# Attention scores of two heads: one zero-padded matmul, or two 64-row matmuls

## The chip, the cores and the metric

The program runs on one core of a Trainium2 chip. The metric is the device time of one execution in microseconds (us), less is better. TensorE (PE) multiplies, VectorE (DVE), ScalarE (ACT) and GpSimd (POOL) work elementwise, and SyncE (SP) issues the DMAs. TensorE writes into PSUM, which has eight banks of 512 fp32 columns.

## What is computed

Windowed attention with a distance bias, then a dense block with a squared ReLU, then a mixture of eight experts whose gate goes through eight rounds of normalisation. The part that the change touches is the first product of the attention; cut down:

```
q, k, v: (4, 8, 576, 64)                      # batch, heads, sequence, head size
scores = q @ k.T / 8                          # 64 values are summed for each score
mask: 0 <= query - key < 128
scores = where(mask, scores - slope[head] * distance, -1e9)
attn = exp(scores - max); attn /= sum + 1e-9
x = attn @ v                                  # to (2304, 512)
x = relu(x @ w_in) ** 2 @ w_out               # 512 -> 2048 -> 512
P = balanced(exp(x @ w_gate))                 # (2304, 8)
out = sum over e of P[:, e] * (relu(x @ w1[e]) @ w2[e])
```

## The kernel before

The engines run programs of their own and wait for each other through semaphores; no scheduler orders the work. The order is a list of events that every engine's program walks through (`alone_events`, L287, and `window_events`, L300). The program has four stages.

- **Ahead of the loop** the attention of batch 0 runs alone. Here all tiles that two steps share are doubled (n = 2), and q and k stay in fp32 (`plain`).
- **The loop** has three passes. Pass w computes the dense block of batch w and, between its matmuls, the attention of batch w + 1. The dense block is cut into 64 groups: eight rounds of four groups of layer 1 (L636, mostly 12 matmuls each) and four of layer 2 (L643; the first has 21 matmuls, the second 3, the others 12). Here q and k are split into a high and a low fp32r part, and a score is the sum of three products (n = 1).
- Then the dense block of batch 3 without attention, and then the experts (L704 and L760).

A batch's attention takes the heads in four pairs (c = 0 to 3). Of a pair, 576 positions make four tiles of 128 and a tail of 64, so that a batch has 4 x 5 = 20 steps. One **slot** holds step j's scores (`scores`, L601), the transposes of step j - 2's probabilities (`transpose_p`, L612) and the product of step j - 3 with the values (`attend`, L627). A query tile needs its own key tile and the one before it; only the first of a pair (t = 0) has one key tile. In the loop slot j stands behind group 2 * (4 + j + j // 5) + 1.

Before a pair's scores, its k and q have to lie with the head's 64 values on the partitions. That is done in three **rounds** (`transpose_round`, L563): round 0 transposes four tiles of k (L572), round 1 four tiles of q, round 2 both tails (L576). All write bank 3 (t_ps). ACT copies the bank out (`round_hi`, L824; in the loop this is the high part), then DVE (`round_lo`, L1003; in the loop the low part), which adds to the semaphore t_lo, for which the next round waits. The two heads of a pair fill partitions 0 to 63 and 64 to 127. The keys (kzh, kzl, and kz0 ahead of the loop) are kept twice as wide, one half for each head, with zeros on the other head's partitions. So one matmul with all 128 rows and 2 x 256 columns gives both heads' scores, in one bank (s_ps: bank 0, and 4 where n = 2). DVE reads them from there (`biased`, L1028), adds the bias, and notes the negative maximum; that raises neg_done, after which the bank is free. ACT takes the exponentials (L854), DVE divides by the sums (L1065), and only then can slot j + 2 transpose them.

In the loop the rounds of pair 0 stand behind groups 3, 5 and 8, those of the next pairs behind the group n of slot 4, 9 or 14 (behind that slot), n + 2 and n + 5. SP loads a pair's k and q when the transposes of the pair before are done.

## Time and profile before

| | |
|---|---|
| median of 3 runs | 2166.37 us (2164.35 to 2172.43) |
| the profiled execution | 2173.03 us |
| its span, first to last instruction | 2171.2 us |
| TensorE busy with matmuls | 2113.9 us (97% of the span) |
| VectorE, ScalarE, GpSimd busy | 1362.2, 588.7, 976.9 us |
| ahead of the loop | 0 to 70.5 us |
| the three passes | 70.5 to 219.9, to 367.7, to 512.4 us |
| dense block of batch 3 | to 634.4 us |
| experts | to the end |

A row of the profile names the line, the engine and the instruction, then what it writes and what it reads, with the shape as rows * columns of the array, then partitions x elements. The ends of matmuls are modelled: of a single matmul the duration includes its way through the array, so two that follow each other overlap in the rows. What a matmul costs is read from the distance between two starts. Where a row stands for several instructions (x4), its duration runs from the first start to the last end. "idle before <- who" is the time in which the engine stood still and what released it.

### The profile page before, as it was taken

To read this page: it belongs to the slowest core of one execution; us is meant where nothing else is said; L and a number is where in the kernel's file an instruction comes from. 1 tells how busy PE (TensorE), PEld (TensorE's weight loads), DVE (VectorE), ACT (ScalarE), POOL (GpSimd) and SP (SyncE) were. 2 spreads that over 40 slices of the span, in tenths; PEclk is the share of its full clock that TensorE was granted. 3 is DMA by queue.
4 is the path that set the end of the run, shared out by engine and by line. 5 is a ranking of instruction groups with operands and counts; after the bars stand their busy time and mean duration, and the time that the engine had idled before them with its cause. 6 is when DMAs were issued, how large, how long until landed. Compare 5 with 4: busy or idle time off the path is not lost.

```text
span 2171.2 us, 39510 instructions
## 1 busy us (share of the span) xinstructions
PE 2113.9 (97%) x13270; PEld 1909.8 (88%) x13270; DVE 1362.2 (63%) x3012; ACT 588.7 (27%) x1609; POOL 976.9 (45%) x680
## 2 busy tenths in 40 slices
PE   7899999999899899999999999999999999999999
PEld 4799898889888799899899899889989989989988
DVE  7566675675556766666666666666666666666665
ACT  5565564564421121111111111211111111111111
POOL 3122222224444354554554554665455455455451
PEclk9999999999999999999999999999999999999999
DMA  5232333322210111111111111112111111111111
GB/s 124 63 82 65 93 87 82 87 71 74 69 49 30 39 40 49 40 49 48 39 48 43 43 48 39 48 41 91 50 39 48 48 39 48 43 44 48 39 48 53
DMA packets 165123, 121.05 MB, mean 56 GB/s; under 512 B 64400, under 2 KB 129936, under 8 KB 165008
## 3 DMA queue, kind: packets, MB, share of 16 engines
q1 hardware_dynamic: 165008, 119.59, 19.4%
q8 instruction: 63, 1.03, 0.2%
q14 instruction: 52, 0.43, 0.1%
HBM read 114.84 MB, written 4.72 MB: 55 GB/s over the span
## 4 chain that ended last, share of the span: by engine, by line
PE 91%; DVE 6%; ACT 2%; issue 2%; DMA 0%; SPq 0%; DVEq 0%; ACTq 0%
PE bank L760 35%; PE bank L704 33%; PE bank L643 9%; PE bank L636 8%; PE bank L601 2%; PE bank L627 1%; PE bank L612 1%; DVE g1l L1077 1%; DVE relu L1108 1%; DVE xl L1091 1%; DVE row L1142 1%; ACT prob L854 1%; PE bank L572 0%; DVE acc L1219 0%; DVE prob L1065 0%
## 5 line engine op out<-in xcount | busy, mean ns | idle before, releaser
L1226 DVE SCALAR_TENSOR_TENSOR acc<-bank,gate,acc 128x512 f32<-128x512 f32 x531 | 398.5, 751 | 285.5 <-PE bank L760 283.6
L704 PE MATMUL bank<-xh,eh 128*128 128x288 f32 x1792 | 532.2, 297 | 0.5 <-DVE u L1192 0.5
L704 PE MATMUL bank<-xl,eh 128*128 128x288 f32 x1792 | 530.7, 296 | 0.0
L704 PE MATMUL bank<-xh,el 128*128 128x288 f32 x1792 | 528.6, 295 | 0.0
L760 PE MATMUL bank<-fh,gh 128*128 128x512 f32 x1152 | 450.9, 391 | 0.7 <-DVE acc L1219 0.4
L760 PE MATMUL bank<-fh,gl 128*128 128x512 f32 x1152 | 450.7, 391 | 0.0
L760 PE MATMUL bank<-fl,gh 128*128 128x512 f32 x1152 | 450.6, 391 | 0.0
L704 PEld LDWEIGHTS bank<-xh,eh 128*128 128x128 f32 x1792 | 338.0, 189 | 3.3 <-DVE u L1192 0.7
L704 PEld LDWEIGHTS bank<-xl,eh 128*128 128x128 f32 x1792 | 338.2, 189 | 2.6
L704 PEld LDWEIGHTS bank<-xh,el 128*128 128x128 f32 x1792 | 339.1, 189 | 0.0
L483 POOL TENSOR_TENSOR wl<-stage,wh 128x512 fp32r<-128x512 f32 x120 | 159.1, 1326 | 380.1 <-ACT wh L822 380.1
L529 POOL TENSOR_TENSOR ew<-a,ew 128x256 f32<-128x256 f32 x64 | 47.3, 740 | 507.6 <-DMA ew<-in_moe_w_dram 489.5
L1184 DVE SCALAR_TENSOR_TENSOR gl<-bank,gh 128x288 fp32r<-128x288 f32 x512 | 220.8, 452 | 76.4 <-ACT gh L941 61.0
L822 ACT ACTIVATE p<-bank 128x288 f32<-128x288 f32 x128 | 52.3, 409 | 784.5 <-PE bank L704 784.5
L538 POOL TENSOR_TENSOR el<-ew,eh 128x1792 fp32r<-128x1792 f32 x64 | 259.6, 4056 | 11.5 <-POOL eh L536 11.5
L760 PEld LDWEIGHTS bank<-fh,gl 128*128 128x128 f32 x1152 | 216.9, 188 | 45.8
L760 PEld LDWEIGHTS bank<-fh,gh 128*128 128x128 f32 x1152 | 216.8, 188 | 45.4 <-DVE acc L1226 0.9
L760 PEld LDWEIGHTS bank<-fl,gh 128*128 128x128 f32 x1152 | 216.9, 188 | 43.5
L636 PE MATMUL bank<-xr,wh 128*128 (+1 forms) x1024 | 213.2, 302 | 4.7 <-issue 3.7
L636 PEld LDWEIGHTS bank<-xr,wh 128*128 128x128 f32 x1024 | 166.3, 191 | 9.1 <-issue 8.3
L643 PE MATMUL bank<-g1h,wh 128*128 128x288 f32 x512 | 160.1, 313 | 14.6 <-DVE g1l L1077 14.5
L542 POOL TENSOR_TENSOR fl<-fw,fh 128x1024 fp32r<-128x1024 f32 x64 | 154.9, 2420 | 11.5 <-POOL fh L540 11.5
(128 smaller groups left out, 2987.9 us busy)
## 6 DMA issues: line engine op xcount, KB each, us to landing
fw<-in_moe_w_dram SPq DMA_DIRECT2D x64, 512.0 KB, 3.6
stage<-in_moe_w_in_dram SPq DMA_DIRECT2D x64, 256.0 KB, 3.0
stage<-in_moe_w_out_dram SPq DMA_DIRECT2D x64, 256.0 KB, 2.7
ew<-in_moe_w_dram SPq DMA_DIRECT2D x64, 256.0 KB, 2.8
a<-in_moe_w_dram SPq DMA_DIRECT2D x64, 128.0 KB, 2.6
ew<-in_moe_w_dram SPq DMA_DIRECT2D x64, 128.0 KB, 2.8
k_raw<-in_k_dram SPq DMA_DIRECT2D x32, 128.0 KB, 2.6
q_raw<-in_q_dram SPq DMA_DIRECT2D x32, 128.0 KB, 2.5
```

The source lines that it names most:

```text
L483: pool.tensor_tensor(wl[s][:, i, :], stage[:, i % 2, :], f(wh[s][:, i, :]), ALU.subtract).then_inc(w_split, 1)
L529: pool.tensor_tensor(raw[:, S1, :, :], a21[r][:, :, :], raw[:, A22, :, :], ALU.add).then_inc(e_chain, 1)
L538: pool.tensor_tensor(el[r][:, :, :, :], raw[:, :, :, :], low, ALU.subtract).then_inc(e_split, 1)
L542: pool.tensor_tensor(fl[r][:, :, :], fw[r][:, :, :], f(fh[r][:, :, :]), ALU.subtract).then_inc(f_split, 1)
L601: last = pe.matmul(o, x[:, t * P:(t + 1) * P], y[:, :, n0:(t + 1) * P], start=(i == 0), stop=(i == len(products) - 1))
L636: last = pe.matmul(ps[:, 0:nt], w[s][:, kc, c * P:(c + 1) * P], xx[:, kc, at], start=(kc == 0 and w is wh and xx is hi), stop=(kc == KC - ...
L643: last = pe.matmul(ys[m % len(ys)][:, 0:BH], w[s][:, KC + c, m * P:(m + 1) * P], x[:, c, :], start=(c == 0 and w is wh and x is g1h), stop ...
L704: done = pe.matmul(ps[:, 0:BH], w[r][:, a, kc, :], x[:, j, b, kc, :], start=(first and kc == 0 and w is eh and x is xh), stop=(kc == 1 and ...
L760: done = pe.matmul(z_ps[t % 3][:, :], x[:, c, at], w[r][:, c, :], start=(c == 0 and x is ghf and w is fh), stop=(c == 1 and x is glf))
L822: return act.activation(o, i, ACT.Copy, scale=scale)
L1184: return dve.scalar_tensor_tensor(out=gl[:, f2, j, n2, :], in0=ps, scalar=0.0, in1=f(gh[:, f2, j, n2, :]), op0=ALU.max, op1=ALU.subtract)
L1226: dve.scalar_tensor_tensor(out=z, in0=ps, scalar=weight, in1=z, op0=ALU.mult, op1=ALU.add).then_inc(z_free, 1)
```

## The change

The keys are kept once (kTh, kTl, kT0), each head on its own 64 partitions and without zeros. A score product becomes two matmuls that read 64 partitions each, one a head, with half as many columns. They write two banks: ahead of the loop banks 0 and 4 for head 0 and banks 6 and 7 for head 1, in the loop bank 0 and bank 3. Bank 3 is also the one that the rounds write, so in the loop a round has to wait until DVE has read the scores of head 1 (neg_done), and the rounds stand in other places: behind groups 3, 5 and 7 for pair 0, and behind n + 1, n + 2 and n + 5 for the others. The scores of slot 0 wait for three rounds, those of a later pair's first tile for two and of its second tile (before: its fifth) for all three. Copies of k go over 128 partitions in one instruction. Ahead of the loop ACT alone copies k out, DVE only steps the semaphore; the clearing of the padded keys goes.

```diff
-        kz0 = sb("kz0", [P, 2, 2, QT * P], fp32, placed["qT0"])
+        kT0 = sb("kT0", [P, 2, QT * P], fp32, placed["qT0"])
...
-        kzh = sb("kzh", [P, 2, QT * P], fp32r, placed["qTl"])
-        kzl = sb("kzl", [P, 2, QT * P], fp32r, placed["kzh"])
-        v_sb = sb("v_sb", [P, 2, QT, 2 * D], fp32, placed["kzl"])
+        kTh = sb("kTh", [P, QT * P], fp32r, placed["qTl"])
+        kTl = sb("kTl", [P, QT * P], fp32r, placed["kTh"])
+        v_sb = sb("v_sb", [P, 2, QT, 2 * D], fp32, placed["kTl"])
...
-        s_ps, pT_ps = [bank[0], bank[4]], [bank[1], bank[5]]
+        pT_ps = [bank[1], bank[5]]
         o_ps, t_ps = bank[2], bank[3]
...
+        def s_ps(j, n, h):
+            if h == 0:
+                return bank[4 * (j % n)][:, 0:2 * P]
+            return bank[3 if n == 1 else 6 + j % 2][:, 0:2 * P]
...
             after = {n: [] for n in range(len(groups))}
-            apart = (0, 2, 5)
+            apart = (1, 2, 5)
             if with_attention:
                 for r in range(ROUNDS):
-                    after[3 + apart[r]].append(("round", 0, r))
+                    after[3 + 2 * r].append(("round", 0, r))
                 after[0] += [("v", 0), ("v", 1)]
...
             pool.memset(ones[:, :], 1.0).then_inc(ones_ready, 1)
-            for z in (kzh[:], kzl[:], qTh[:, FULL * P:], qTl[:, FULL * P:]):
+            for z in (kTh[:, FULL * P:], kTl[:, FULL * P:], qTh[:, FULL * P:], qTl[:, FULL * P:]):
                 pool.memset(f(z), 0.0).then_inc(zeros_later, 1)
...
             pe.wait_ge(ident_ready, 1)
-            pe.wait_ge(zeros_ready, 3)
-            def transpose_round(b, c, r):
+            pe.wait_ge(zeros_ready, 2)
+            def transpose_round(b, c, r, before=0):
                 if r < 2:
...
                     wait_alone(pe, t_lo, b * (ROUNDS * KC) + (ROUNDS * c + r))
+                    if plain(b):
+                        pe.wait_ge(t_hi, ROUNDS * c + r)
+                if before:
+                    wait_alone(pe, neg_done, b * STEPS + before)
                 if r < 2:
...
                 if t == 0:
-                    pe.wait_ge(t_lo, b * (ROUNDS * KC) + ROUNDS * c + 2)
-                if t == FULL:
+                    pe.wait_ge(t_lo, b * (ROUNDS * KC) + ROUNDS * c + (2 if n > 1 or c else 3))
+                if t == (FULL if n > 1 else 1):
                     pe.wait_ge(t_lo, b * (ROUNDS * KC) + ROUNDS * (c + 1))
+                if plain(b) and t in (0, FULL):
+                    pe.wait_ge(t_hi, ROUNDS * c + (2 if t == 0 else 3))
                 bank_wait(neg_done, b, j, n)
-                o = s_ps[j % n][:, :].rearrange("p (h k) -> p h k", h=2)[:, :, k0:]
                 n0 = (t - 1) * P + k0
                 if plain(b):
-                    products = ((qT0[:, s, :], kz0[:, s, :, :]),)
+                    products = ((qT0[:, s, :], kT0[:, s, :]),)
                 else:
-                    products = ((qTh, kzh), (qTh, kzl), (qTl, kzh))
+                    products = ((qTh, kTh), (qTh, kTl), (qTl, kTh))
                 for i, (x, y) in enumerate(products):
-                    last = pe.matmul(o, x[:, t * P:(t + 1) * P], y[:, :, n0:(t + 1) * P],
-                                     start=(i == 0), stop=(i == len(products) - 1))
+                    for h in range(2):
+                        d = slice(h * D, (h + 1) * D)
+                        last = pe.matmul(s_ps(j, n, h)[:, k0:], x[d, t * P:(t + 1) * P], y[d, n0:(t + 1) * P],
+                                         start=(i == 0), stop=(i == len(products) - 1))
                 last.then_inc(s_done, 1)
...
                     if what == "round":
-                        transpose_round(b, *a)
+                        transpose_round(b, *a, 0 if n > 1 or a[0] == 0 else a[0] * QT + (a[1] == 2))
                     if what == "slot":
...
                 s = c % n
+                act.wait_ge(t_done, b * (ROUNDS * KC) + (ROUNDS * c + r + 1))
                 if plain(b):
-                    act.wait_ge(t_done, b * (ROUNDS * KC) + (ROUNDS * c + r + 1))
                     if r == 1:
                         act.sem_inc(t_hi, 1)
-                        return
-                    o, i = (slice(0, FULL * P), slice(0, FULL * P)) if r == 0 else (slice(FULL * P, S), slice(TAIL, 2 * TAIL))
-                    for h in range(2 if r else 1):
-                        d = slice(h * D, (h + 1) * D)
-                        last = copy(kz0[d, s, h, o], t_ps[d, i])
-                    last.then_inc(t_hi, 1)
+                    elif r == 0:
+                        copy(kT0[:, s, 0:FULL * P], t_ps[:, :]).then_inc(t_hi, 1)
+                    else:
+                        copy(kT0[:, s, FULL * P:S], t_ps[:, TAIL:2 * TAIL]).then_inc(t_hi, 1)
                     return
-                act.wait_ge(t_done, b * (ROUNDS * KC) + (ROUNDS * c + r + 1))
-                if r == 1:
+                if r == 0:
+                    last = copy(kTh[:, 0:FULL * P], t_ps[:, :])
+                elif r == 1:
                     last = copy(qTh[:, 0:FULL * P], t_ps[:, :], SCALE)
-                if r == 2:
+                else:
                     copy(qTh[:, FULL * P:S], t_ps[:, 0:TAIL], SCALE)
-                if r != 1:
-                    o, i = (slice(0, FULL * P), slice(0, FULL * P)) if r == 0 else (slice(FULL * P, S), slice(TAIL, 2 * TAIL))
-                    for h in range(2):
-                        last = copy(kzh[h * D:(h + 1) * D, h, o], t_ps[h * D:(h + 1) * D, i])
+                    last = copy(kTh[:, FULL * P:S], t_ps[:, TAIL:2 * TAIL])
                 last.then_inc(t_hi, 1)
...
             dve.memset(qT0[:, :, FULL * P:], 0.0).then_inc(zeros_ready, 1)
-            for r in range(2):
-                dve.memset(kz0[:, r, :, :], 0.0).then_inc(zeros_ready, 1)
+            dve.memset(kT0[:, :, FULL * P:], 0.0).then_inc(zeros_ready, 1)
             dve.wait_ge(dist_ready, 1)
...
-                    dve.wait_ge(t_done if r == 1 else t_hi, b * (ROUNDS * KC) + (ROUNDS * c + r + 1))
                     if r == 0:
-                        last = dve.tensor_copy(kz0[D:2 * D, s, 1, 0:FULL * P], t_ps[D:2 * D, :])
-                    else:
-                        at = slice(0, FULL * P) if r == 1 else slice(FULL * P, S)
-                        last = dve.tensor_scalar(qT0[:, s, at], t_ps[:, 0:FULL * P if r == 1 else TAIL],
-                                                 SCALE, None, ALU.mult)
-                    last.then_inc(t_lo, 1)
+                        dve.sem_inc(t_lo, 1)
+                        return
+                    dve.wait_ge(t_done if r == 1 else t_hi, ROUNDS * c + r + 1)
+                    at = slice(0, FULL * P) if r == 1 else slice(FULL * P, S)
+                    dve.tensor_scalar(qT0[:, s, at], t_ps[:, 0:FULL * P if r == 1 else TAIL],
+                                      SCALE, None, ALU.mult).then_inc(t_lo, 1)
                     return
                 dve.wait_ge(t_hi, b * (ROUNDS * KC) + (ROUNDS * c + r + 1))
-                if r == 1:
+                if r == 0:
+                    last = lo(kTl[:, 0:FULL * P], t_ps[:, :], kTh[:, 0:FULL * P])
+                elif r == 1:
                     last = lo(qTl[:, 0:FULL * P], t_ps[:, :], qTh[:, 0:FULL * P], SCALE)
-                if r == 2:
+                else:
                     lo(qTl[:, FULL * P:S], t_ps[:, 0:TAIL], qTh[:, FULL * P:S], SCALE)
-                if r != 1:
-                    o, i = (slice(0, FULL * P), slice(0, FULL * P)) if r == 0 else (slice(FULL * P, S), slice(TAIL, 2 * TAIL))
-                    for h in range(2):
-                        d = slice(h * D, (h + 1) * D)
-                        last = lo(kzl[d, h, o], t_ps[d, i], kzh[d, h, o])
+                    last = lo(kTl[:, FULL * P:S], t_ps[:, TAIL:2 * TAIL], kTh[:, FULL * P:S])
                 last.then_inc(t_lo, 1)
...
                 last = dve.tensor_tensor_reduce(
-                    out=prob[0:nq, j % 2, h, k0:], in0=s_ps[j % n][0:nq, h * 2 * P + k0:(h + 1) * 2 * P],
+                    out=prob[0:nq, j % 2, h, k0:], in0=s_ps(j, n, h)[0:nq, k0:],
                     in1=bias[0:nq, 2 * (j // QT) + h, k0:], scale=-1.0, scalar=3.0e38,
...
```

The instruction streams, at three places. TensorE in the loop, slot 1, the scores and the transposes behind them. Before:

```order
L601 MATMUL bank<-kzh,qTh 128x512 [waits neg_done]
L601 MATMUL bank<-kzl,qTh 128x512
L601 MATMUL bank<-kzh,qTl 128x512
L612 MATMUL bank<-ident,prob 128x128 [waits pT_out,norm_done]
L612 MATMUL bank<-ident,prob 128x128 x3
```

Of the change:

```order
L615 MATMUL bank<-kTh,qTh 128x256 [waits neg_done]
L615 MATMUL bank<-kTh,qTh 128x256
L615 MATMUL bank<-kTl,qTh 128x256 x2
L615 MATMUL bank<-kTh,qTl 128x256 x2
L626 MATMUL bank<-ident,prob 128x128 [waits pT_out,norm_done]
L626 MATMUL bank<-ident,prob 128x128 x3
```

Three matmuls of 512 columns have become six of 256, the two heads in turn.

TensorE in the loop, around the first round of pair 1 (k_raw; q_raw is the second round's). Before:

```order
L627 MATMUL bank<-pT,v_sb 64x128 [waits x_lo,pT_out]
L627 MATMUL bank<-pT,v_sb 64x128 x3
L565 REGISTER_ALU
L572 MATMUL bank<-ident,k_raw 128x128 [waits k_in,t_lo]
L572 MATMUL bank<-ident,k_raw 128x128 x3
L666 REGISTER_ALU
L636 MATMUL bank<-xr,wh_51 128x288 [waits relu_done]
```

Of the change:

```order
L650 MATMUL bank<-xr,wl_53 128x288
L572 REGISTER_ALU
L268 REGISTER_ALU [waits k_in,t_lo]
L583 MATMUL bank<-ident,k_raw 128x128 [waits neg_done]
L583 MATMUL bank<-ident,k_raw 128x128 x3
L680 REGISTER_ALU
L650 MATMUL bank<-xr,wh_51 128x288 [waits relu_done]
```

The transposes of k have moved from behind slot 4's product with the values to behind the layer-1 group that follows; the transposes of q stay where they were, one group on.

DVE at the start of the program. Before:

```order
L989 MEMSET qT_55 128x2x128
L991 MEMSET kz_56 128x1280 x2
L994 TENSOR_SCALAR bias<-prob 128x256 [waits dist_ready]
L994 TENSOR_SCALAR bias<-prob 128x256 x7
L1009 COPY kz_56<-bank 64x512 [waits bias_ready,t_hi]
L1012 TENSOR_SCALAR qT_55<-bank 128x512 [waits t_done]
```

Of the change:

```order
L999 MEMSET qT_55 128x2x128
L1000 MEMSET kT_56 128x2x128
L1003 TENSOR_SCALAR bias<-prob 128x256 [waits dist_ready]
L1003 TENSOR_SCALAR bias<-prob 128x256 x7
L1021 TENSOR_SCALAR qT_55<-bank 128x512 [waits bias_ready,t_done]
```

Two clearings of 1280 columns have become one of 256, and the copy of k is no longer DVE's.

## Rows read from the trace of the kernel before

**Rows 1.** The page's chain of work that ended last, shares by engine.
```profile
PE 91%; DVE 6%; ACT 2%; issue 2%; DMA 0%; SPq 0%; DVEq 0%; ACTq 0%
```

**Rows 2.** Stretches: window, length, busy us (instructions) of each engine, clock, DMA.
```profile
0.00:70.50 70.50, 50.20 (x296) 28.00 (x296) 49.80 (x203) 39.93 (x133) 19.96 (x32) 0.97 0.41 97
...
219.90:367.70 147.80, 144.28 (x1084) 132.26 (x1084) 95.06 (x300) 82.40 (x240) 42.18 (x32) 0.99 0.32 82
```

**Rows 3.** Timeline (start, duration, engine, line, instruction) of TensorE, a wide slot in the loop.
```profile
252.63 0.40 PE L601 MATMUL bank<-kzl,qTh 128*128 128x512 f32 x1
252.86 0.39 PE L601 MATMUL bank<-kzh,qTl 128*128 128x512 f32 x1
...
253.99 0.53 PE L636 MATMUL bank<-xr,wh 128*128 x2
254.36 0.29 PE L636 MATMUL bank<-xr,wl 128*128 x1
254.49 0.43 PE L636 MATMUL bank<-xr,wh 128*128 x2
```

**Rows 4.** Timeline of TensorE, a slot whose transposes have 64 rows.
```profile
301.46 0.39 PE L601 MATMUL bank<-kzh,qTl 128*128 128x512 f32 x1
301.78 0.46 PE L612 MATMUL bank<-ident,prob 64*128 64x64 f32 x4
```

**Rows 5.** Timeline of TensorE, a narrow slot (one key tile).
```profile
266.83 0.28 PE L601 MATMUL bank<-kzh,qTh 128*128 128x256 f32 x1
266.95 0.28 PE L601 MATMUL bank<-kzl,qTh 128*128 128x256 f32 x1
```

**Rows 6.** Timeline of TensorE, the gate's matmuls on four column tiles.
```profile
645.52 4.09 PE L777 MATMUL bank<-acc,wgz 128*32 128x288 f32 x64
```

**Rows 7.** Timeline of all engines, rounds 0 and 1 of a pass's first pair.
```profile
229.85 1.18 ACT L822 ACTIVATE kzh<-bank 64x512 fp32r<-64x512 f32 x2
...
231.06 1.39 DVE L1001 SCALAR_TENSOR_TENSOR kzl<-bank,kzh 64x512 fp32r<-64x512 f32 x2 [0.63 <-ACT kzh L822]
...
231.44 0.29 PE L643 MATMUL bank<-g1h,wl 128*128 128x288 f32 x1
...
232.60 0.63 PE L572 MATMUL bank<-ident,q_raw 128*128 128x128 f32 x4 [0.86 <-DVE kzl L1001]
```

**Rows 8.** Timeline of all engines, rounds 0 and 1 of the second pair (pair 1).
```profile
259.06 0.66 PE L572 MATMUL bank<-ident,k_raw 128*128 128x128 f32 x4
...
261.33 0.41 ACT L917 ACTIVATE relu<-bank 128x288 f32<-128x288 f32 x1 [0.38 <-PE bank L636]
...
261.97 0.62 ACT L822 ACTIVATE wh<-stage 128x512 fp32r<-128x512 f32 x1
...
262.71 0.60 PE L572 MATMUL bank<-ident,q_raw 128*128 128x128 f32 x4
...
265.13 0.40 PE L643 MATMUL bank<-g1h,wh 128*128 128x288 f32 x1 [0.23 <-DVE g1l L1077]
```

**Rows 9.** Timeline of DVE, round 2 of the third pair (pair 2).
```profile
301.02 0.45 DVE L1001 SCALAR_TENSOR_TENSOR kzl<-bank,kzh 64x64 fp32r<-64x64 f32 x2
```

**Rows 10.** Line L994 (ns min/median/max), and the timeline of all engines, near the start.
```profile
L994 DVE TENSOR_SCALAR bias<-prob x8: 273/279/2023, 3.7 to 7.1; 128x256 f32<-128x256 f32 x8
...
8.29 1.09 PE L572 MATMUL bank<-ident,q_raw 128*128 128x128 f32 x4 [2.40 <-DVE kz L1009]
...
8.94 0.60 SPq L360 DMA_DIRECT2D v_sb<-in_v_dram  x1
```

**Rows 11.** Chain of waits ahead of the loop: start, length, what.
```profile
10.81 0.37 SPq L358
...
15.37 1.71 PE bank L601 x2
...
26.09 1.05 PE bank L601 x2
...
49.19 2.00 PE bank L601 x2
```

## The prediction

> **What bounds the kernel now.** I read the chain of waits first: 91% of it is TensorE [rows 1]. Then the stretches: in one pass of the loop that holds the attention (three passes) TensorE is busy for 144.28 of 147.80 us, in the stage ahead of the loop for 50.20 of 70.50 [rows 2]. So in the loop each TensorE start that moves later costs its own length. Ahead of it, DVE, ACT and TensorE take turns, and only what is on their chain counts. The change touches nothing after the third pass: at most some 512 of 2171 us are in play.
>
> **Score matmuls in the loop.** A slot has three matmuls of 512 columns, 0.23 apart (252.63 to 252.86), 0.70 in all [rows 3]; where a query tile has one key tile they have 256 columns and are 0.12 apart, 0.36 in all [rows 5]. Afterwards there are six of 64 rows and half as many columns, for two heads in turn. The trace of before has no such pair. The nearest rows are matmuls on different column tiles: 64 of 288 columns take 4.09, 0.06 each [rows 6], against 0.13 for one 288-column matmul on the whole array (254.36 to 254.49 [rows 3]), so several run at once. I take it that row tiles overlap in the same way: a pair of 256 columns then takes 0.12, as one such matmul does now.
>
> Against that stand two changes of tiling in each slot. (a) The change itself: from the third 128-row score matmul to the first 64-row transpose 0.32 pass, not 0.23 [rows 4]: 0.09. (b) The first weight load behind a change isn't hidden: behind the column-tiled matmuls of attend the first two 128-row matmuls take 0.37 (253.99 to 254.36), two later ones would take 2 x 0.13: 0.11 [rows 3]. Into transposes it is less: four take 0.66 behind attend and 0.60 behind a layer-1 matmul [rows 8]: 0.06. By these:
> - a wide slot followed by 128-row transposes (12 in a pass): 0.09 + 0.11 + 3 x 0.12 + 0.09 + 0.06 = 0.71 for 0.70, so +0.01 each;
> - the three wide slots whose transposes have 64 rows themselves: no way out is paid, and the way in that the old code paid (0.09 and about 0.05) goes: 0.56 for 0.84, -0.28 each;
> - the narrow slots: 128 columns stream in about 0.06, less than the load (0.11), which sets the pace: 0.09 + 0.11 + 2 x 0.11 + 0.06 + 0.15 = 0.63 for 0.36, +0.27, three times, and +0.34 for slot 0, which is followed by a layer matmul; slot 1 for the same reason +0.06.
> Sum of a pass: 0.12 - 0.84 + 0.81 + 0.34 + 0.06 = +0.5; three passes **+1.5 us**. Halving the streamed columns is paid back by drains and loads.
>
> The Trainium skill (TensorE: Matmul & The Clock Gate, Part 3, table of measured speed-ups) gives 3.07 for four row tiles, less than four. As an estimate from that page, a pair would keep 77% of the overlap, which adds some 5 us to the sum; no run here shows it.
>
> **Copies of the keys, and the rounds, in the loop.** A round's key copy falls from two 64-partition instructions each on ACT (1.18) and DVE (1.39) to one each, half of that [rows 7].
> - First pair of a pass: ACT starts at 229.85, would be done at 230.45, and DVE, free by then, at 231.2 (half of 1.18 and of 1.39). TensorE's matmul of 231.44 is followed 0.13 later by the transposes of q, at 231.57, and not at 232.60, where they wait for that copy [rows 7]: -1.03, three times, **-3.1**.
> - Pairs 1 and 3: the transposes of k now come one layer-1 group later (bank 3 holds head 1's scores until DVE has read them) and those of q stay, so one group of some 1.6 us lies between them, not two. Queued ahead on ACT are that group's relu and the copy of a square (0.64 from 261.33 to 261.97) and a weight copy (0.62) [rows 8]. From 259.06 the group's 12 matmuls take 0.24 + 10 x 0.13, and k's last transpose starts at about 261.1. Then: relu at 260.95, the weight copy done at 262.2, key copy to 262.7, DVE's part to 263.45, transposes of q at 263.6 where TensorE could have started them at 262.8. That is a new stall of 0.8. TensorE's wait ahead of 265.13, 0.23 idle for a square that DVE delivers late [rows 8], then goes, because the stall comes before it. Net 0.8 - 0.23, so about +0.5, six times: **+3.0**. Bounds: 0 (ACT serves the copy at once) and +0.8 each.
> - Pair 2: groups of layer 2 give ACT less to do; +0.1. The third round has to be copied one slot sooner (the wait moved from tile 4 to tile 1). In pair 2 DVE's part ends at 301.47 now [rows 9], 0.25 sooner with one copy fewer on ACT and DVE, while the scores started at 300.99, two starts of 0.23 before the row of 301.46 [rows 4]: +0.2 to +0.3. In pairs 1 and 3 ACT has no relu there and I count nothing. Leaving the transposes of k between two layer groups and not behind attend costs 0.05 a round (one more unhidden load of 0.11, one of 0.06 saved). Together +0.45 a pass, **+1.3**.
> - The new waits for head 1's scores (round 0 and round 2) find them read: DVE reads within a microsecond, the group between takes 1.6. Nothing; if not, up to 0.5 each, 18 times, which is a rival below.
> Loop: +1.5 - 3.1 + 3.0 + 1.3 = **+2.7**.
>
> **Ahead of the loop.** DVE no longer clears 2 x 1280 columns and POOL clears two times 1280 fewer, which it now does while DVE's first bias instruction takes 2.02, where the median is 0.28 [rows 10]. DVE's copy of k (some 0.7, as half of the 1.39 [rows 7]) is gone too. Both stand ahead of q's transposes at 8.29 [rows 10]: by 1.7 + 0.7 they could start some 2 us sooner, once q has landed. But the next loads of k are issued by SP behind those of v, whose last issue starts at 8.94 and takes 0.60 [rows 10]; the k load is issued at 10.81 now [rows 11] and can go to 9.54, so it moves by 1.27 at most. I take -1.25. The second matmul pair behind it is on the chain with 1.71 [rows 11]: half of the columns and the two changes of tiling, -0.3. Another stands there with 2.00, about twice the 1.05 of the one at 26.09 [rows 11], so at the lower of the two levels: -0.5. In three places scores are on the chain with that 1.05, and DVE's normalised tile is next to be late: 0 to -0.3 each, I take -0.15. ACT's tail copy is one instruction and not two: -0.2. Sum -1.25 - 0.3 - 0.5 - 0.45 - 0.2 = **-2.7**; bounds -1 and -5. Elsewhere the chain there runs over DVE, ACT and the transposes, and faster scores only wait longer.
>
> **Sum.** +2.7 - 2.7 = 0.0. The profiled run took 2173.03 (span 2171.2), the median is 2166.37; the terms are differences and carry over: **2166 us**. About 0.5% (11 us) is what a measurement of this kernel can tell from no change.
>
> **Rivals.**
> 1. *Row tiles do not overlap.* Six matmuls of 0.12 then take 0.72 in a wide slot, +0.36, in 48 slots +17; narrow slots have six loads of 0.11, +0.33, 12 times +4; ahead of the loop +2. 2166 + 23 = **2189**, slower. It decides at 0.17 for a pair instead of 0.12. Against it: column tiles overlap fully [rows 6]. For it: no row shows two row tiles at once.
> 2. *Loads inside the row-tiled stretch are not hidden.* Each later pair costs 0.11 more: 2 x 0.11 x 48 = +10, **2176**. The Trainium skill (TensorE: Matmul & The Clock Gate, Part 3, what overlaps and what doesn't) says a load overlaps running matmuls only where its row group differs. Against it speaks the row of four 64-row transposes, all on one row group, in 0.46 [rows 4], where loads in the open would add to each.
> 3. *The copies get in the way*: the new waits for scores in bank 3 and for the third round bind (0.5 in 18 rounds), the stall of pairs 1 and 3 is 1.3 and not 0.8: +9 + 3, **2178**. For it: DVE is busy for 95.06 of 147.80 [rows 2] and serves in order. Against it: the layer groups give it 1.6 us.
> 4. *Entering and leaving cost nothing here*, because the two row tiles drain one behind the other's back: -0.35 in 57 slots, -20, with -4 ahead of the loop for the clock kept up: **2144**, faster. Against it: [rows 4] is a change into 64 rows and has the 0.09.
> 5. *The change does not do what it says* (the 64-row form is executed as full 128 rows, each matmul alone): the same as rival 1.
>
> **Chances.** Forecast 0.66 (2158 to 2173: the stalls at their bounds, the start between -1 and -5, and a stretch of lower clock more or less at a loop boundary). Rival 1 and 5 together 0.13, rival 2 0.06, rival 3 0.06, rival 4, whole or in part, 0.09. The range 2157 to 2180 leaves out rival 1 and most of rival 4. Faster by over 0.5% (under 2155.5) 0.10, slower (over 2177.2) 0.16, within 0.74.
>
> **What would show it.** Score matmuls in pairs that start within 0.01 of each other, pairs 0.12 apart, and some 0.09 more before the first and behind the last; if all six are 0.12 apart, rival 1 holds. No wait in front of the transposes of q in a pass's first pair; one of about 0.8 in pairs 1 and 3. Transposes of q before 7.1 at the start, the loop from about 67.8 instead of 70.5, passes about 1 us longer than now. I am wrong if pairs lie much closer than 0.12, if the 0.11 for the load is missing, or if the rounds wait for neg_done.

## The result, and the profile after

The changed kernel takes **2171.8 us** (median of 20 executions, 2168.5 to 2175.6) where the kernel before takes 2166.7 (2163.0 to 2172.4): ratio 1.0022, 95% interval 1.0013 to 1.0030, so 4.9 us more (2.8 to 6.5). The forecast was 2166.0, no difference. The time lies within the range, but the difference is real, and it is a loss. (A ratio, here and below, compares with executions of the kernel before that were taken beside it. It isn't the quotient of the two medians: in run 6 it is 1.0033 where the medians give 1.0016.) The profiled execution took 2173.73 us with a span of 2171.7, nearly the 2171.2 of before; one profile of each, laid side by side, doesn't show where the time is.

Most of what the forecast said of the rows came true. The chain of waits is still TensorE's:

```profile
PE 92%; DVE 5%; ACT 1%; issue 1%; SPq 0%; DMA 0%; DVEq 0%; ACTq 0%
```

A wide slot in the loop (timeline of TensorE; a row of x2 is one pair, head 0 and head 1), beside [rows 3]:

```profile
251.10 0.29 PE L657 MATMUL bank<-g1h,wl 128*128 128x288 f32 x1
251.33 0.38 PE L615 MATMUL bank<-kTh,qTh 64*128 64x256 f32 x2
251.55 0.28 PE L615 MATMUL bank<-kTl,qTh 64*128 64x256 f32 x2
251.67 0.28 PE L615 MATMUL bank<-kTh,qTl 64*128 64x256 f32 x2
251.88 0.66 PE L626 MATMUL bank<-ident,prob 128*128 128x128 f32 x4
```

Two row tiles run at once: in a row of x2 they start some 0.005 apart, and the third pair follows the second after 0.12, as one 256-column matmul did. Ahead of the first pair stand 0.23 instead of 0.13 (the change of tiling), behind it 0.22 (the load in the open), behind the last 0.21. Slots with 64-row transposes and narrow slots, beside [rows 4, 5]:

```profile
301.13 0.39 PE L615 MATMUL bank<-kTh,qTh 64*128 64x256 f32 x2
301.32 0.32 PE L615 MATMUL bank<-kTl,qTh 64*128 64x256 f32 x2
301.44 0.31 PE L615 MATMUL bank<-kTh,qTl 64*128 64x256 f32 x2
301.56 0.40 PE L626 MATMUL bank<-ident,prob 64*128 64x64 f32 x4
...
266.31 0.33 PE L615 MATMUL bank<-kTh,qTh 64*128 64x128 f32 x2
266.48 0.27 PE L615 MATMUL bank<-kTl,qTh 64*128 64x128 f32 x2
266.59 0.28 PE L615 MATMUL bank<-kTh,qTl 64*128 64x128 f32 x2
266.79 0.66 PE L626 MATMUL bank<-ident,prob 128*128 128x128 f32 x4
```

From a 64-row pair into 64-row transposes only 0.12 pass: no way out is paid. The rounds, beside [rows 7, 8]. In pair 0 (the first five rows) the transposes of q follow without a wait. In pair 1 ACT has a relu, a square and a weight copy ahead of the key copy; DVE is done at 262.28, and TensorE waits 0.80 for it:

```profile
229.38 0.58 ACT L836 ACTIVATE kTh<-bank 128x512 fp32r<-128x512 f32 x1
229.99 0.69 DVE L1010 SCALAR_TENSOR_TENSOR kTl<-bank,kTh 128x512 fp32r<-128x512 f32 x1
...
231.12 0.60 PE L583 MATMUL bank<-ident,q_raw 128*128 128x128 f32 x4
...
259.61 0.60 PE L583 MATMUL bank<-ident,k_raw 128*128 128x128 f32 x4
...
260.44 0.62 ACT L836 ACTIVATE wh<-stage 128x512 fp32r<-128x512 f32 x1
...
260.96 0.59 ACT L836 ACTIVATE kTh<-bank 128x512 fp32r<-128x512 f32 x1
...
261.59 0.69 DVE L1010 SCALAR_TENSOR_TENSOR kTl<-bank,kTh 128x512 fp32r<-128x512 f32 x1 [0.51 <-ACT kTh L836]
...
262.57 0.63 PE L583 MATMUL bank<-ident,q_raw 128*128 128x128 f32 x4 [0.80 <-DVE kTl L1010]
```

The start (timeline of all engines), beside [rows 10, 11]. DVE's first bias instruction no longer stretches to 2.02 (line L1003 has a maximum of 0.841), so q's transposes start at 6.40 and not at 8.29. But k of the next pair is issued only at 9.67 to 10.77, behind v, and its transposes wait 3.30 for it; in before they start at 14.29. Of 1.9 us won, 0.8 are left:

```profile
6.40 1.09 PE L583 MATMUL bank<-ident,q_raw 128*128 128x128 f32 x4 [0.88 <-DMA q_raw<-in_q_dram]
...
8.94 0.60 SPq L366 DMA_DIRECT2D v_sb<-in_v_dram  x1
...
9.67 1.06 SPq L364 DMA_DIRECT2D k_raw<-in_k_dram  x2
...
10.77 0.60 SPq L366 DMA_DIRECT2D k_raw<-in_k_dram  x1
...
13.50 1.09 PE L583 MATMUL bank<-ident,k_raw 128*128 128x128 f32 x4 [3.30 <-DMA k_raw<-in_k_dram]
```

The stretches, beside [rows 2]. The granted clock is the third figure from the end, here 0.90, 0.80 and 1.00; 1.00 is the upper level (2.4 GHz), half of it the lower one:

```profile
0.00:70.80 70.80, 49.56 (x336) 31.47 (x336) 42.72 (x198) 39.23 (x129) 18.04 (x32) 0.90 0.41 97
27.00:78.00 51.00, 39.96 (x291) 28.11 (x288) 30.36 (x143) 29.99 (x101) 10.67 (x11) 0.80 0.28 71
220.90:368.10 147.20, 143.11 (x1144) 129.50 (x1144) 90.05 (x292) 78.98 (x232) 41.62 (x32) 1.00 0.32 83
```

The loop starts at 70.83, not at 67.8; ahead of it the clock is 0.90, where before has 0.97.

Both figures are too high. The trace of before has its first record of the clock at 18.4, that of the change at 25.8, and the view counts 1.00 until then, though the matmuls run at the lower level. Four transposes of probabilities, in the chain of waits of before, then of the change:

```profile
20.16 0.65 PE bank L612 x4
```
```profile
25.00 1.02 PE bank L626 x4
```

So of the time ahead of the loop the change spends 40 us at the lower level (25.8, and 14.3 of the later stretches) and before 23 (18.4 and 4.3).

### The profile page after: what moved, and what is told of

Same layout as the page of the kernel before. It is cut to its first block, busy times and chain, and to the rows that moved or that the text cites. A ratio compares the mean times of both kernels' runs of the same rounds, so it can differ in the third digit from the quotient of the medians.

```text
span 2171.7 us, 39932 instructions
## 1 busy us (share of the span) xinstructions
PE 2114.6 (97%) x13490; PEld 1909.6 (88%) x13490; DVE 1342.1 (62%) x2983; ACT 577.7 (27%) x1581; POOL 973.4 (45%) x680
## 4 chain that ended last, share of the span: by engine, by line
PE 92%; DVE 5%; ACT 1%; issue 1%; SPq 0%; DMA 0%; DVEq 0%; ACTq 0%
PE bank L774 35%; PE bank L718 33%; PE bank L657 9%; PE bank L650 9%; PE bank L641 2%; PE bank L626 2%; PE bank L615 2%; DVE xl L1097 1%; DVE row L1148 1%; PE bank L583 1%; DVE relu L1114 1%; DVE g1l L1083 0%; DVE prob L1041 0%; ACT prob L864 0%; DVE acc L1225 0%
```

## Experiments

**Theory A.** The new loop costs what the forecast says. Ahead of it the 64-row scores leave TensorE idle for longer, the granted clock falls more often, and that takes back the earlier start. **Rivals:** all of the loss is in the loop (B); the earlier start lowers the clock (C).

Loop starts and pass lengths below are read from the first layer-1 matmul of each pass. A mean clock is the mean over all executions of a kernel of the granted clock of each; a clock of a stretch, and the microseconds at the lower level, are those of the one profiled execution.

**1. Ahead of the loop alone** (`ahead_only`): as after, but in the loop

```diff
-                    products = ((qTh, kTh), (qTh, kTl), (qTl, kTh))
+                    products = ((qTh, kzh), (qTh, kzl), (qTl, kzh))
...
-            apart = (1, 2, 5)
+            apart = (0, 2, 5)
```

with the copies, waits, bank and clearing of before. Expected:

> Only the stage ahead of the loop is changed (64-row score matmuls, keys unpadded, ACT alone copies k); the loop keeps the padded keys, the 128-row matmuls and the old places of the rounds. Theory A (the shorter score matmuls leave TensorE idle for more of this stage, so it is granted the lower clock for longer, and that takes back what the earlier start gave): in the trace of the changed kernel 40 of the first 71 us are at the lower level, in that of before 23, and the loop starts at 70.8 as against 70.5; so 0 to +3 us against the kernel before, and a loop start at 70 to 73. Rival B (the forecast's sum for this stage was right, and all of the loss is in the loop): -2.7 us, loop start at about 68.

Measured: 2166.03, ratio 0.9996 (0.9987 to 1.0005), so -0.9 us (-2.8 to +1.1). That is below A's 0 to +3, and the interval excludes neither A nor B's -2.7. The loop start, 72.07, is as A says. It is the profile with the lowest clock ahead of the loop, 0.76 from 27 to 78 us:

```profile
27.00:78.00 51.00, 41.77 (x292) 28.57 (x291) 31.93 (x141) 30.06 (x102) 10.63 (x11) 0.76 0.27 67
```

Since the sum with the next run didn't come to 4.9, it was run again:

> The change ahead of the loop alone, once more and on another chip. Its first result does not add up with the others: the new loop costs 0.75 a pass (2.3) in every profile, the whole change 4.9, so the part ahead of the loop should cost some 2.6, but it measured 2166.03 against 2167.49. Theory A (its low clock is a matter of chance from execution to execution, more often than with the old scores): this time clock 0.989 to 0.990 and 2168 to 2170, and in the profile again 13 us or more at the lower level before 78 us. Rival (with the old loop behind it the stage is better off, and the clock of the whole change has a second cause in the loop): 0.991 and 2165.5 to 2166.5 again.

Measured: 2168.16, ratio 1.0000 (0.9991 to 1.0009), loop start 69.19, 0.87 from 27 to 78. The mean clock of its executions is 0.9907 (first run 0.9908), between the 0.9926 of before and the 0.9893 of the change. A's time (2168 to 2170) and its 13 us at the lower level (13.7) were met, its clock (0.989 to 0.990) was not; of the rival, the clock was met and the time was not. So the stage alone brings nothing that can be measured (-0.9 and 0.0 us; -2.7 is outside the second interval), and with the new loop behind it the clock is a little lower still.

**2. The loop alone** (`loop_only`): as after, but ahead of the loop the padded `kz0`, its clearing and copies, and

```diff
-                    products = ((qT0[:, s, :], kT0[:, s, :]),)
+                    pe.matmul(o, qT0[:, s, t * P:(t + 1) * P], kz0[:, s, :, n0:(t + 1) * P],
+                              start=True, stop=True).then_inc(s_done, 1)
```

> Only the loop is changed; the stage ahead of it keeps padded keys, their clearing, and one 128-row score matmul a step. Theory A: the loop costs what the forecast's sum for it says, +2.7 us, since passes 2 and 3 in the trace of the changed kernel are 1.1 (with the one stretch of lower clock of before at 219.8 taken out) and 0.7 us longer than before, and the stage ahead +2. Rival B: the loop costs the whole +4.9, above all through its new wait for the transposes of q in pairs 1 and 3 (0.93 instead of 0.8, six times) and something that the two traces do not show; then +4.5 to +5.

Measured: 2169.03, ratio 1.0006 (0.9997 to 1.0015), mean clock 0.9924 as before. A's +2.7 lies within the interval (-0.6 to +3.3); B's +4.5 is out. The passes settle it. These are the ones that run wholly at the upper level, without those of `apart135` (other places of the rounds) and of `after_fill` (run 3); one of the five at 145.25 is `apart025`:

| | old loop | new loop |
|---|---|---|
| pass 1 | 146.56 | 147.29, 147.33 |
| pass 2 | 146.39, 146.42, 146.48, 146.53, 146.65 | 146.99, 147.25, 147.46, 147.47 |
| pass 3 | 144.49 to 144.53 (6 profiles) | 145.25 to 145.26 (5 profiles) |

So some 0.75 a pass, 2.3 us in three.

**3. More work for TensorE, as added instructions** (`after_fill`):

```diff
+                if plain(b):
+                    for i in range(4):
+                        pe.transpose(pT_ps[j % n][:, i % 4 * P:(i % 4 + 1) * P], ident[:, :], ident[:, :])
                 wait_alone(pe, norm_done, b * STEPS + (j + 1))
```

> The changed kernel, and ahead of the loop four more 128x128 transposes of the identity in each step, into the bank that the step's own transposes overwrite, just before TensorE waits for the normalised probabilities: work without use where it stands idle for 1.0 to 1.7 us in each step. Theory A (idle time ahead of the loop costs clock): the stage ends earlier, loop start at 67 to 69 instead of 70.8, 2 to 4 us less than the changed kernel, about 2168 where the kernel before takes 2166.7. Rival B (the clock there plays no part): the extra work is hidden at best, 2172, and later where it sticks out, up to 0.2 in each of 20 steps, 2176.

Measured: 2175.95, ratio 1.0043 (1.0029 to 1.0056), the time of B. Clock and loop start do what A says (1.00 from 27 to 78, mean clock 0.9920, loop start 68.59), but this kernel doesn't test A's price: passes 2 and 3 last 151.99 and 149.48, 4.7 and 4.2 more than in after, though nothing in the loop was changed (at these two boundaries it is also at the lower level for 6.8 and 3.4 us). At both boundaries a second wait (2.23 and 2.42) stands behind the first, without a releaser in the profile; the boundary at 216:

```profile
216.17 0.40 PE L653 MATMUL bank<-xr,wh 128*128 x1 [2.11 <-issue]
218.80 0.61 PE L653 MATMUL bank<-xr,wh 128*128 x1 [2.23 <-issue]
```

160 more TensorE instructions (80 transposes and their loads) moved the loop's code; that this is the cause is my guess and wasn't tried. The next experiment keeps the number of instructions.

**4. The same work, no instruction more** (`after_wide`):

```diff
+                        if plain(b):
+                            full = bank[4 * (j % n) if h == 0 else 6 + j % 2]
+                            last = pe.matmul(full[:, :].rearrange("p (r k) -> p r k", r=2)[:, :, k0:],
+                                             x[d, t * P:(t + 1) * P],
+                                             y[d, n0:(t + 1) * P].unsqueeze(1).to_broadcast([D, 2, (t + 1) * P - n0]),
+                                             start=True, stop=True)
+                            continue
```

(`plain` holds ahead of the loop only; each trace has 336 matmuls ahead of the loop.) 

> The changed kernel, but ahead of the loop each 64-row score matmul streams its keys twice (512 columns into the whole bank, the second 256 never read), so TensorE is as long at the scores as with padded keys, with not one instruction more or less. Theory A (what the change loses is TensorE's clock ahead of the loop, because TensorE has less to do there): mean granted clock back from 0.989 to 0.992 or more, at most 10 us at the lower level before 77 us instead of 20 to 31, loop start at 66 to 69, and 2167 to 2169 instead of 2171.8, although each step has 0.25 more work. Rival B (the clock is lower for another reason, such as the earlier start or the phase of the loads): clock 0.989 as before, and the extra columns cost 0.3 to 1 us: 2172 to 2173.

Measured: 2168.84, ratio 1.0012 (1.0003 to 1.0021); mean clock 0.9922, loop start 68.22. A holds in every number, B in none. **TensorE streams twice the columns at these scores, and the kernel takes 1.5 and 2.9 us less than the two medians of the change.** The intervals of the ratios overlap, but the means of the executions (2168.8 against 2171.5 and 2171.8) differ by 2.7 with a standard error of 0.6 from the first, and the clock goes with them. The clock from 27 to 78, this kernel, then before (its second profile, below):

```profile
27.00:78.00 51.00, 41.49 (x305) 26.78 (x301) 32.33 (x142) 31.13 (x102) 11.39 (x12) 0.93 0.31 79
```
```profile
27.00:78.00 51.00, 42.29 (x285) 27.58 (x285) 32.94 (x147) 32.07 (x107) 11.49 (x12) 0.93 0.33 81
```

**5. The same with the old loop** (`ahead_wide_oldloop`, the edits of 1 and 4):

> The same twice-streamed scores ahead of the loop, with the old loop (padded keys, 128-row matmuls, old places of the rounds). Theory A with the loop's cost of 0.75 a pass (pass 3 at full clock: 144.50 and 144.53 with the old loop, 145.25 and 145.26 with the new): 2.3 us less than the run above, and 2 us less than the change ahead of the loop alone (2166.0), so 2163 to 2165, below both kernels. Rival B: 2166.5, clock 0.991.

Measured: 2165.18, ratio 0.9999 (0.9989 to 1.0008), mean clock 0.9927, loop start 68.38. The median is 0.2 above A's band and 3.7 below run 4, but against before it shows no gain; the clock is A's, not B's 0.991.

**6. The change once more, and before once more** (`after_again`, `before_again`; no edit):

> The changed kernel once more, on the chip of the runs beside it. Theory A: median 2171 to 2173, mean granted clock 0.989 to 0.990 over its executions where the kernel before shows 0.992 to 0.993, its span at an equal granted clock within 1 us of that of before, and in this second profile again 15 us or more at the lower level before 77 us. Rival B (the loss is time at full clock, and the low clock of the first profile was chance): the same clock as the kernel before and still 4 to 5 us more.

> The kernel before, for a second profile. Theory A: less than 15 us at the lower level before 77 us (10.2 in the first one, 20 to 31 in three profiles with short scores ahead of the loop); pass 3 at full clock 144.5. Rival (the stretches are chance and not the kernel's): 20 us or more.

Measured: after 2170.38, ratio 1.0033 (1.0019 to 1.0046), mean clock 0.9894 beside 0.9929 of before on that chip. The median is 0.6 below A's band; clock and lower level (17 us between 33.7 and 50.7) are A's. The loop starts at 69.92. Before: 0.93 from 27 to 78 (6.8 us at the lower level), **loop start 68.33, not 70.54**, pass 3 144.50; both are A's. The profile that the forecast was made from was itself a late one.

**7. The rounds' places.** `apart025` puts k's transposes back behind the slot; `apart135` puts q's one group later, with (1, 3, 5) in this line:

```diff
-            apart = (1, 2, 5)
+            apart = (0, 2, 5)
```

> The changed kernel, but the transposes of k of pairs 1 to 3 back in their old place directly behind the slot (one layer-1 group earlier), now behind a wait for head 1's scores in bank 3. If the new stall of 0.93 in front of the transposes of q (six times) is what the loop's loss is made of: it goes, -0.8 x 6, less a wait for DVE behind attend that I put at 0 to 0.4 nine times (the slot's transposes and attend take 1.2 us, about what DVE needs for both heads' scores), so 2167 to 2170 and the loop's loss of some 2.5 us is gone. Rival: DVE is later than that (it has the group's squares queued ahead), and the wait behind the slot costs as much as the stall: 2171 to 2173.

> The changed kernel, but the transposes of q of pairs 1 to 3 one layer group later (n + 3), so that two groups lie between them and those of k, as before. Theory A (one group of 1.6 us is too short for ACT's and DVE's copy): the wait of 0.93 in front of them goes, but the pair's first scores now follow one group behind q's transposes and wait for q's copy instead, 0.4 to 0.9; pass 3 between 144.7 and 145.3, total 2169.5 to 2172. Rival: the copies of q fit into that group, the wait is gone altogether, pass 3 at 143.7 to 144.2 and the total at 2167 to 2168.5: then the change's loss in the loop is the placement alone, and the 64-row matmuls gain there.

Measured: `apart025` 2171.64, ratio 1.0018 (1.0009 to 1.0028), pass 3 145.25, the same as in after to 0.01; I expected 2167 to 2170. The wait only moved, to k's transposes behind attend, three times a pass:

```profile
406.42 0.63 PE L583 MATMUL bank<-ident,k_raw 128*128 128x128 f32 x4 [0.64 <-DVE negmax L1041]
```

My 0 to 0.4 for it was low; the rival held. `apart135`: 2175.47, ratio 1.0049 (1.0035 to 1.0063), slower than both and outside both expectations. The pair's first scores now wait for q's copy, 1.1 in pairs 1 and 3, where my 0.4 to 0.9 was low, and 0.3 in pair 2:

```profile
414.32 0.33 PE L615 MATMUL bank<-kTh,qTh 64*128 64x128 f32 x2 [1.11 <-DVE qTl L1010]
...
443.70 0.33 PE L615 MATMUL bank<-kTh,qTh 64*128 64x128 f32 x2 [0.30 <-DVE qTl L1010]
```

So the places of the change are the best of these three; with bank 3 shared, one of the two waits has to be paid.

**8. The earlier start** (`after_slowclear`):

```diff
-            for z in (kTh[:, FULL * P:], kTl[:, FULL * P:], qTh[:, FULL * P:], qTl[:, FULL * P:]):
+            for z in (kTh[:], kTl[:], qTh[:], qTl[:]):
```

> The changed kernel, but POOL clears all 640 columns of kTh, kTl, qTh and qTl (2560 in all, about what the kernel before clears) and not 128 of each. It delays DVE's biases and with them q's first transposes, which start at 6.40 in the changed kernel and at 7.60 where the loop (and so the clearing) is the old one. It asks why the granted clock of the changed kernel (0.989) is lower than with the change ahead of the loop alone (0.991). Theory C (the earlier first transposes leave TensorE idle longer until the next k lands at 13.5, and that starts the stage on the lower level): q's transposes at 7.6, those of pair 1's k still at 13.5, mean clock back to 0.991, median 2169 to 2170. Rival (the start plays no part; only the shorter scores do): the same 0.989, 2170 to 2172, and the earlier start was worth nothing either way.

Measured: 2172.69, ratio 1.0026 (1.0016 to 1.0036), mean clock 0.9888: the clock of the rival, the time 0.7 above it. q's transposes start at 7.52, those of k at 13.56 (after: 13.50). C falls: the start plays no part in the clock, and the first 1.1 us of the earlier start were worth 0.06.

**9. A try at a faster kernel** (`wide_tail_oldloop`: run 5, and in the last three steps ahead of the loop)

```diff
+                if plain(b) and j >= STEPS - 3:
+                    pe.matmul(pT_ps[j % n][:, :].rearrange("p (r k) -> p r k", r=4), ident[:, :],
+                              ident[:, :].unsqueeze(1).to_broadcast([P, 4, P]), start=True, stop=True)
```

> The 64-row scores ahead of the loop streaming their keys twice, the old loop, and in the last three steps ahead of the loop one more 512-column matmul of the identity before TensorE waits for the normalised probabilities. In both kernels with twice-streamed scores TensorE falls to the lower level at 67, as the attention of batch 0 runs out, and 5.2 to 5.5 us of that lie in the first pass. Theory A: with the idle time of 62 to 67 filled, this stretch goes or is halved: first pass 146.4 to 147.7 instead of 148.96, clock 0.993 to 0.994, total 2163 to 2165 where the kernel before takes 2166.9. Rival: waits of 1.2 and 1.4 between the last products with the values remain and decide it: no change, 2165 to 2166.

Measured: 2166.21, ratio 0.9994 (0.9985 to 1.0002). In the profile the lower level from 67 on is gone, as A said, and pass 1 takes 146.56:

```profile
27.00:78.00 51.00, 44.84 (x333) 28.10 (x332) 33.49 (x146) 33.28 (x106) 11.97 (x12) 1.00 0.34 86
```

The mean clock is 0.9936, the highest of all, but the median missed A's 2163 to 2165 by 1.2; a gain over before isn't shown.

**All profiles together.** Scores "short" are single 64-row pairs ahead of the loop, "long" those of before or streamed twice:

| profile | scores | clock 27 to 78 | loop start |
|---|---|---|---|
| after, after_again | short | 0.80, 0.83 | 70.83, 69.92 |
| ahead_only, again | short | 0.76, 0.87 | 72.07, 69.19 |
| apart025, apart135, after_slowclear | short | 0.83, 0.87, 0.87 | 70.66, 68.42, 68.97 |
| before, before_again | long | 0.90, 0.93 | 70.54, 68.33 |
| loop_only, after_wide | long | 1.00, 0.93 | 67.13, 68.22 |
| ahead_wide_oldloop, wide_tail_oldloop | long | 0.93, 1.00 | 68.38, 67.93 |

Every short clock is below every long one; the loop starts overlap. The means are 0.83 and 0.95 (17 and 5 us at the lower level), the mean loop starts 70.0 and 68.4. `after_fill`, short scores with the added work of run 3, has 1.00 and 68.59. The first rise to the upper level comes between 16.6 and 26.5 with short scores and between 17.4 and 19.1 with long ones; no granted clock given here counts what is lost before it.

**All executions together.** Over 216 executions of all these kernels a straight line with one slope and a level for each kernel gives 1.34 us for each 0.001 of mean clock (standard error 0.07). At an equal clock the change, both runs together, then lies 0.1 above before (standard error 0.4), which is A's expectation in run 6; `ahead_only`, both runs, 2.3 below (0.35), `loop_only` 1.3 above (0.4), `after_wide` 1.1 above (0.4). This is read from scatter and not from an edit, and a microsecond at the lower level need not cost the same in each stage (with the slope of `ahead_only` itself, 0.9, its 2.3 are some 1.5).

## Why the prediction was wrong

**Right: the loop, in most of its terms to a few hundredths.** Set against `ahead_only` in pass 3, where both run at the upper level, each slot and round measures (forecast in brackets): wide slot followed by 128-row transposes 0.00 (+0.01), narrow slot +0.27 (+0.27), slot 0 +0.32 (+0.34), slot 1 +0.06 (+0.06), slot with 64-row transposes -0.24 to -0.30 (-0.28), pair 0 -1.00 (-1.03), a moved k round +0.05 (+0.05), pair 2's wait +0.24 (+0.1). The sum was 0.9 a pass and is 0.75: 2.3 us against 2.7.

In pairs 1 and 3 the net is the forecast's +0.5 by luck. The new stall measures +0.97 from start to start (0.8), and the wait for a late square that goes in exchange is worth 0.45 (0.23). Both forecasts took the idle time of a row, and the starts move by more than that. The wait that goes, as it stands in `ahead_only` (starts 0.52 and 0.24 apart, where 0.13 is the rule):

```profile
409.66 0.29 PE L665 MATMUL bank<-g1h,wl 128*128 128x288 f32 x1
410.18 0.40 PE L665 MATMUL bank<-g1h,wh 128*128 128x288 f32 x1 [0.23 <-DVE g1l L1094]
410.42 0.30 PE L665 MATMUL bank<-g1l,wh 128*128 128x288 f32 x1
```

(The prediction also rounds 0.8 - 0.23 down to 0.5, and its sum for rival 4 comes to 2142, not 2144; neither changes the verdict.) Of the +0.2 to +0.3 for the third round of pair 2 some 0.05 is there: the slot that would wait for it gives -0.24, the two like it -0.29 and -0.30.

**Rivals 1, 2, 4 and 5** are out by the rows of the wide slot: pairs overlap whole, their loads are hidden after the first (0.12 between the second and the third pair), and entering and leaving cost 0.1 each. The estimate from the Trainium skill (TensorE: Matmul & The Clock Gate, Part 3, table of measured speed-ups) that a pair keeps 77% of the overlap isn't borne out: the pair takes the 0.12 of one matmul. Nor is that part's rule borne out that a load overlaps running matmuls only where its row group differs: here each pair uses both row groups again, and the third pair follows the second after the same 0.12. Of rival 3, the stall was mis-sized by 0.17; the new wait for head 1's scores doesn't bind in the places of the change, and does at 0.64 one group earlier.

**Wrong: the step "Ahead of the loop", -2.7.** What failed in it is above all a term that it doesn't have: the clock.
- *The clock, put at nothing.* I priced one step at the lower level as a saving and did not ask whether less work lowers the level of all the others. It does (run 4): without one instruction changed in number, more columns brought the mean clock from 0.989 to 0.992 and the median from 2170.4 (on the same chip) to 2168.8. The change's mean clock is 0.9893 where that of before is 0.9921 to 0.9929. The difference of 0.0033 to their mean is some 14 us more at the lower level in an execution, and by the line through all executions 4.5 us.
- *Scores on the chain, -0.3 - 0.5 - 0.45.* These took the chain of one profile. The chain of before has scores at the upper level in three places, with 1.05 each (1.06 the last). In the chain of the change all four places with scores lie at the lower level (up to 25.8, and 36.1 to 46.3), with up to 1.16. So at the upper level they did leave the chain, and the lower level put them back on it:

```profile
21.11 1.07 PE bank L615 x4
...
24.27 0.73 PE bank L615 x4
...
38.35 0.73 PE bank L615 x4
...
41.18 1.16 PE bank L615 x4
```

  Elsewhere the work that goes turns into waiting, as the forecast said it would, and this is the idle time that it did not price. A step ahead of the loop had two 128-row matmuls and now has four of 64 rows:

```profile
58.24 0.63 PE L612 MATMUL bank<-ident,prob 128*128 128x128 f32 x4 [0.82 <-DVE prob L1065]
...
59.17 1.13 PE L601 MATMUL bank<-kz,qT 128*128 128x512 f32 x2
60.60 0.63 PE L612 MATMUL bank<-ident,prob 128*128 128x128 f32 x4 [0.30 <-DVE prob L1065]
```
```profile
58.42 0.70 PE L615 MATMUL bank<-kT,qT 64*128 64x256 f32 x4
60.13 0.63 PE L626 MATMUL bank<-ident,prob 128*128 128x128 f32 x4 [1.00 <-DVE prob L1071]
...
62.48 0.30 PE L626 MATMUL bank<-ident,prob 128*128 128x128 f32 x1 [0.73 <-DVE prob L1071]
```

  (timeline of TensorE, before in its second profile, then after, both at the upper level). 0.4 us of work a step goes, and a step takes 2.36 before (58.24 to 60.60) and 2.35 after (60.13 to 62.48), by DVE and ACT.
- *The k load, -1.25.* It was seen that SP's queue bounds it, and its first issue did move by 1.14 (10.81 to 9.67), but the transposes only by 0.79 (14.29 to 13.50): the last issue moved by 1.00, and the transfer behind it took 2.59, where before has 2.38. The chain of waits of after:

```profile
10.77 2.59 DMA k_raw<-in_k_dram
```

  Run 8 shows that what was won beyond the queue is worth nothing.

What the term for ACT's tail copy (-0.2) was worth, no run shows.

**The sum.** At an equal clock the forecast's 0.0 holds for the whole change (+0.1, standard error 0.4), with some of its -2.7 ahead of the loop (-2.3, or -1.5 by the other slope) and most of its +2.7 in the loop (+1.3; +2.3 by the passes). The 4.9, whose interval reaches from 2.8 to 6.5, are then nearly all clock. By the profiles, the loop starts 1.6 later on average (70.0 against 68.4) instead of 2.7 earlier, and the new loop adds 2.3: 3.9 of the 4.9.

**Open** is where all of the clock is lost. Of the 14 us, 12 lie between 27 and 78 in the averages of the profiles. The rest may be further drops: in 5 of 8 profiles with the new loop the lower level appears at a boundary of two passes, in 1 of 6 with the old one, and `ahead_only` has a higher mean clock than the whole change (0.991 against 0.989). In the loop 3.4 us at the lower level cost some 1.6 (pass 3 takes 146.85 in run 8 and 145.25 without them). No run sets this apart.

A second mistake is one of method: 70.5 stood as *the* loop start of before. It is one execution's; in the second profile it was 68.33. A term of -1 to -5 us was set against a number that moves by 2 us by itself.

## What to carry to other kernels

- A matmul that is shortened where TensorE waits for other engines anyway gained nothing there and cost clock for what came next. Before an edit that takes work from a half-idle TensorE, look at the granted clock of that stretch; if it is already below 1.00 (0.90 and 0.93 here), give the clock a term in the sum, and test with an equal number of instructions.
- Where TensorE is the bound, the terms can be added from start-to-start distances to a few hundredths. Splitting a matmul by rows with half the columns brings nothing at this size: what the overlap gives (0.35 in a slot), two changes of tiling and a load in the open take.
- A wait costs more than its row's idle time: 0.97 for an idle 0.80, 0.45 for an idle 0.23. Take the distance between starts.
- For an effect of 0.2%, read every execution's granted clock, not one profile's times, and compare the kernels at an equal clock too.

## What the runs showed that I had not expected

- Twice the columns at the scores ahead of the loop made the kernel faster (2168.8 against 2170.4 and 2171.8), through the clock.
- With 160 useless TensorE instructions ahead of the loop, two later passes took 4.7 and 4.2 us more; at their boundaries a wait of 2.2 and 2.4 us with no releaser appeared. Why is open.
- POOL's clearing stretched the DVE instruction beside it: to 2.47 us with 2816 columns cleared (`ahead_only`) and 2.55 with 2560 (`after_slowclear`, which differs from after in nothing else), where 512 columns leave 0.84 in after and 0.40 in `loop_only`. DVE's own two clearings of 1.1 us each cost nothing: with them (`loop_only`) and without (after) the eight biases end at 5.55.
